# Top-32 attention and two expert stages on one core: mask by clipped distance on ScalarE and one GpSimd subtraction, weight splits on GpSimd

## The reference

```python
top_k = 32
scale = 1.0 / np.sqrt(D)                      # D = 64
scores = scale * np.matmul(q, k.transpose(0, 1, 3, 2))
kth = np.partition(scores, -top_k, axis=-1)[..., -top_k:-top_k + 1]
scores = np.where(scores >= kth, scores, -1000000000.0)
scores = scores - np.max(scores, axis=-1, keepdims=True)
attn = np.exp(scores)
attn = attn / (np.sum(attn, axis=-1, keepdims=True) + 1e-09)
out = np.matmul(attn, v)
...
rms = np.sqrt(np.mean(x * x, axis=-1, keepdims=True) + 1e-06)
xn = x / rms * rms_g
g = xn @ w_gate                               # w_gate, w_val: 512 x 1536
out = (g / (1 + np.exp(-g)) * (xn @ w_val)) @ w_out
```

## Time and profile before

| | us |
|---|---|
| median of 3 runs | 741.94 |
| span of the profiled execution | 741.7 |
| PE busy | 686.1 (93%) |
| DVE busy | 478.9 (65%) |
| ACT busy | 270.4 (36%) |
| POOL busy | 281.5 (38%) |

### The profile page before, as it was taken

One profiled execution on the slowest core, in us unless ns is written; L12 is line 12 of the kernel. 1 busy time (PEld: TensorE's weight loads), 2 busy tenths in 40 slices (PEclk: granted clock), 3 DMA queues, 4 the chain that ended last, 5 costly groups with the idle time before them and its releaser, 6 DMA issues.

```text
span 741.7 us, 10642 instructions
## 1 busy us (share of the span) xinstructions
PE 686.1 (93%) x3862; PEld 557.7 (75%) x3862; DVE 478.9 (65%) x1090; ACT 270.4 (36%) x545; POOL 281.5 (38%) x233
## 2 busy tenths in 40 slices
PE   5696789999999999999999999999994999999994
PEld 3574667588687578688688688687653999999994
DVE  3999979989979968979979979972211011111110
ACT  4385565354354354354354354342210011101110
POOL 1556665646455445545546455452000011110002
PEclk9666599999999999999999999999995999999998
DMA  9999000000000000000000000000055677676501
GB/s 186 363 384 263 0 15 1 0 15 1 14 15 1 15 15 1 11 20 1 14 15 1 15 1 0 15 2 15 0 212 166 256 263 259 231 245 234 204 20 34
DMA packets 52908, 65.43 MB, mean 88 GB/s; under 512 B 32058, under 2 KB 32058, under 8 KB 52860
## 3 DMA queue, kind: packets, MB, share of 16 engines
q1 hardware_dynamic: 51116, 60.05, 25.3%
q0 software_dynamic: 1744, 4.76, 1.7%
HBM read 52.89 MB, written 12.30 MB: 88 GB/s over the span
## 4 chain that ended last, share of the span: by engine, by line
PE 81%; DVE 13%; ACT 1%; DMA 1%; issue 1%; POOL 1%; SPq 0%; POOLq 0%; DVEq 0%; ACTq 0%
PE ps L451 13%; PE ps L593 10%; PE ps L607 10%; PE ps L423 10%; PE ps L401 8%; PE ps L440 6%; PE ps L444 6%; PE ps L441 6%; PE ps L414 4%; PE ps L388 3%; DVE w_top L1006 3%; DVE m L1001 3%; DVE w_parts L909 2%; DVE w_top L993 2%; DVE m L982 1%
## 5 line engine op out<-in xcount | busy, mean ns | idle before, releaser
L1116 POOL TENSOR_SCALAR s_ring<-s_ring,m 128x576 f32<-128x576 f32 x72 | 124.3, 1727 | 179.4 <-DVE m L1010 148.2
L423 PEld LDWEIGHTS ps<-arena,pt_ring 128*128 128x128 f32 (+3 forms) x800 | 99.9, 187 | 22.9 <-issue 8.9
L423 PE MATMUL ps<-arena,pt_ring 128*128 128x65 f32 (+3 forms) x800 | 107.6, 274 | 3.8 <-ACT pt_ring L666 3.7
L1006 DVE MATCH_REPLACE8 w_top<-m,w_top 128x576 f32<-128x576 f32 x144 | 105.8, 742 | 0.0
L1118 POOL TENSOR_TENSOR p_ring<-p_ring,s_ring 128x576 f32<-128x576 f32 x72 | 102.0, 1417 | 6.0
L1001 DVE MAX8 m<-w_top 128x8 f32<-128x576 f32 x144 | 101.6, 747 | 0.0
L451 PE MATMUL ps<-wo_space,hid 128*128 128x512 f32 x216 | 95.8, 593 | 0.0
L401 PE MATMUL ps<-arena,q_cols 128*128 128x288 f32 (+1 forms) x320 | 92.4, 444 | 2.1 <-ACT q_cols L666 1.4
L440 PE MATMUL ps<-w_parts,x_hi 128*128 128x512 f32 x216 | 92.3, 428 | 0.9 <-ACT x_hi L666 0.8
L666 ACT ACTIVATE pt_ring<-ps 128x512 f32<-128x512 f32 (+1 forms) x144 | 54.0, 428 | 95.9 <-PE ps L415 95.6
L441 PE MATMUL ps<-w_parts,x_hi 128*128 128x512 f32 x216 | 85.2, 395 | 0.0
(11 more groups left out here) (116 smaller groups left out, 812.1 us busy)
## 6 DMA issues: line engine op xcount, KB each, us to landing
w_loads<-in_moe_w SPq DMA_DIRECT2D x16, 2048.0 KB, 9.0
dispatched_rows<-hid SPq DMA_DIRECT2D x18, 260.0 KB, 7.4
w_loads<-in_moe_w_gate SPq DMA_DIRECT2D x1, 3072.0 KB, 10.8
w_loads<-in_moe_w_val SPq DMA_DIRECT2D x1, 3072.0 KB, 18.6
wo_space<-in_moe_w_out SPq DMA_DIRECT2D x1, 3072.0 KB, 13.6
arena<-dispatched_rows SPq DMA_DIRECT2D x8, 341.2 KB
out_rows<-hid SPq DMA_DIRECT2D x9, 256.0 KB, 5.2
q_space<-in_q SPq DMA_DIRECT2D x8, 256.0 KB, 2.9
```

The source lines that it names most:

```text
L423: last = mm(ao_ps(u % H, r0, r1), pt_ring[0:n, u % 2, j * P + r0:j * P + r1], vs[b][0:n, j, u % H, :], start=(j == 0), stop=(j == KC - 1))
L1006: vec.match_replace(w_top[:, a, :], m8[:, u % 8, i, :], w_top[:, a, :], NEG).then_inc(s["top_step"], 1)
L1116: gp.tensor_scalar(sc, sc, m8[:, n % 8, TOPK // 8 - 1, 7:8], None, ALU.is_ge).then_inc(s["pchain"], 1)
```

## The change

The exponential moves behind the mask. DVE no longer writes the bias; instead it writes, once per pair and after its last maximum, `far` = the 32nd largest times 2^90. ACT computes relu(far - 2^90 * score): zero where the score is at or above the 32nd largest, and a huge number below it. This is done for both units of a pair in the odd step `u0 + 3`. POOL subtracts it from the score (`lowered`), in one instruction where there were two, and writes the exponential's bias for both units of a pair. ACT takes the exponential in place in step `u + 4`, as the first thing of its step (in slot 4 the second, after `ao`), and that now signals `masked`. The factor 1/8 moves from the exponential to the copy of the queries. All 12 weight pieces now go one way: ACT writes `hi`, and POOL does the two scalings and the subtraction.

The diff, cut to its core (the changed file has other line numbers: its exponential is line 766, its relu 793, `far` 999, the weight multiplies 1100 and the subtraction 1112):

```diff
@@ ffn_block (PE)
-                    if m > in_vec(m):
-                        pe.wait_ge(s["w_lo_set"], m - in_vec(m))
-                    if in_vec(m) > 0:
-                        pe.wait_ge(s["w_lo_vec"], 2 * in_vec(m))
+                    pe.wait_ge(s["w_lo_set"], m)
@@ ACT, after the copy of ao and ahead of turned_probs(u)
+                if 0 <= u < NT * H:
+                    act.wait_ge(s["lowered"], u + 1)
+                    act.wait_ge(s["bias_set"], u // 2 + 1)
+                    nc.scalar.activation(p_ring[:, u % PR, :], p_ring[:, u % PR, :], ACT.Exp,
+                                         bias=nbias[:, u % 8:u % 8 + 1]).then_inc(s["masked"], 1)
@@ ACT, copy of the scores
-                        act.wait_ge(s["masked"], n - SR + 1)
+                        act.wait_ge(s["lowered"], n - SR + 1)
@@ ACT, after the copy of x_hi
-                u = n - EXP_LAG
-                if 0 <= u < NT * H:
-                    act.wait_ge(s["bias_set"], u + 1)
-                    if u >= PR:
-                        act.wait_ge(s["pt_done"], u - PR + 1)
-                    nc.scalar.activation(p_ring[:, u % PR, :], s_ring[:, u % SR, :], ACT.Exp,
-                                         bias=nbias[:, u % 8:u % 8 + 1], scale=SCALE).then_inc(s["exp_done"], 1)
+                for u in (n - 3, n - 2) if n % 2 else ():
+                    if 0 <= u < NT * H:
+                        act.wait_ge(s["far_set"], u // 2 + 1)
+                        if u >= PR:
+                            act.wait_ge(s["pt_done"], u - PR + 1)
+                        nc.scalar.activation(p_ring[:, u % PR, :], s_ring[:, u % SR, :], ACT.Relu, scale=-FAR,
+                                             bias=far[:, u % 2:u % 2 + 1]).then_inc(s["marked"], 1)
@@ ACT, weight pieces
-                    for c in half if m not in VEC_PIECES else ():
-                        nc.scalar.activation(raw[:, c, cols], raw[:, c, cols], ACT.Copy, scale=gain[:, c:c + 1]).then_inc(s["w_scaled"], 1)
@@ DVE, beside(n)
-                if m in VEC_PIECES:
...
-                    for c in half:
-                        vec.scalar_tensor_tensor(out=lo[:, c, cols], in0=raw[:, c, cols], scalar=gain[:, c:c + 1],
-                                                 in1=hi[:, c, cols], op0=ALU.mult, op1=ALU.subtract).then_inc(s["w_lo_vec"], 1)
@@ DVE, pair
-                    vec.tensor_scalar(nbias[:, u % 8:u % 8 + 1], m8[:, u % 8, 0, 0:1], -SCALE, None,
-                                      ALU.mult).then_inc(s["bias_set"], 1)
...
+                dve.wait_ge(s["th_set"], u0 + 2)
+                if u0 > 0:
+                    dve.wait_ge(s["marked"], u0)
+                vec.tensor_scalar(far[:].rearrange("p (a w) -> p a w", w=1), m8[:, u0 % 8:u0 % 8 + 2, TOPK // 8 - 1, 7:8], FAR, None,
+                                  ALU.mult).then_inc(s["far_set"], 1)
@@ POOL
-                if 0 <= m < 4 * FB and m not in VEC_PIECES:
-                    pool.wait_ge(s["w_scaled"], 2 * (m - in_vec(m)) + 2)
+                if 0 <= m < 4 * FB:
+                    pool.wait_ge(s["w_hi_set"], 2 * m + 2)
+                    for c in half:
+                        gp.tensor_scalar(raw[:, c, cols], raw[:, c, cols], gain[:, c:c + 1], None, ALU.mult).then_inc(s["w_scaled"], 1)
+                    pool.wait_ge(s["w_scaled"], 2 * m + 2)
                     gp.tensor_tensor(lo[:, half[0]:half[1] + 1, cols], raw[:, half[0]:half[1] + 1, cols],
                                      hi[:, half[0]:half[1] + 1, cols], ALU.subtract).then_inc(s["w_lo_set"], 1)
+                if n < NT * H and n % 2 == 0:
+                    pool.wait_ge(s["th_set"], n + 2)
+                    gp.tensor_scalar(nbias[:, n % 8:n % 8 + 2].rearrange("p (a w) -> p a w", w=1), m8[:, n % 8:n % 8 + 2, 0, 0:1], -1.0, None,
+                                     ALU.mult).then_inc(s["bias_set"], 1)
                 if n < NT * H:
-                    pool.wait_ge(s["th_set"], n + 1)
-                    pool.wait_ge(s["exp_done"], n + 1)
-                    gp.tensor_scalar(sc, sc, m8[:, n % 8, TOPK // 8 - 1, 7:8], None, ALU.is_ge).then_inc(s["pchain"], 1)
-                    pool.wait_ge(s["pchain"], 4 + n + 1)
-                    gp.tensor_tensor(pr, pr, sc, ALU.mult).then_inc(s["masked"], 1)
+                    pr = p_ring[:, n % PR, :]
+                    pool.wait_ge(s["marked"], n + 1)
+                    gp.tensor_tensor(pr, s_ring[:, n % SR, :], pr, ALU.subtract).then_inc(s["lowered"], 1)
```

More of the change, by code:

```diff
@@ L9 @@
+import math
 from contextlib import ExitStack
@@ L29 @@
 LAG = 4
-EXP_LAG = 2
+FAR = 2.0 ** 90
 KEYS_AT = 3
 SPLIT_AT = 6
-VEC_PIECES = (1, 3, 5, 7, 9, 11)
 RANK = 14
@@ L70, in build @@
     assert B == 2 and NT == 9 and MIX == 4 and H == 8 and KL == 64 and 0 < REST <= P
-    assert S % 2 == 0 and FB == 3 and CF == 12 and CD == 4 and C1 == 8
+    assert S % 2 == 0 and math.frexp(SCALE)[0] == 0.5 and FB == 3 and CF == 12 and CD == 4 and C1 == 8
     disp = nc.dram_tensor("dispatched_rows", [TRASH + N, ROW], F32).ap()
@@ L111, in build @@
         nbias = sb("nbias", [P, 8])
+        far = sb("far", [P, 2])
         rden = sb("rden", [P, H])
@@ L190, in build @@
             "disp_zero out_zero id_set z_set pchain achain vchain "
-            "k_turned k_acted k_veced k1_copied w_hi_set w_scaled w_lo_set w_lo_vec "
+            "k_turned k_acted k_veced k1_copied w_hi_set w_scaled w_lo_set "
             "t_full t_free "
-            "s_done s_copied bias_set top_step th_set exp_done masked pt_done pt_copied pv_done "
+            "s_done s_copied top_step th_set far_set bias_set marked lowered masked pt_done pt_copied pv_done "
             "ao_copied normed x_sum pstep rinv_set x_hi_set blk_full tanh_done silu_done val_done out_full out_copied "
@@ L233, in kind_of @@
             return "mix" if t == MIX else 0 if t < MIX else 1
-        def in_vec(m):
-            return sum(p < m for p in VEC_PIECES)
         def split_piece(m):
@@ L695, in q_columns @@
                 pairs = q_cols[:].rearrange("p (g a) n -> p g a n", a=2)
-                copy(pairs[0:64, :, 0, :], turned[0:64]).then_inc(s["achain"], 1)
+                nc.scalar.activation(pairs[0:64, :, 0, :], turned[0:64], ACT.Copy, scale=SCALE).then_inc(s["achain"], 1)
                 act.wait_ge(s["achain"], t + 1)
-                copy(pairs[64:P, :, 1, :], turned[64:P]).then_inc(s["t_free"], 1)
+                nc.scalar.activation(pairs[64:P, :, 1, :], turned[64:P], ACT.Copy, scale=SCALE).then_inc(s["t_free"], 1)
             def hidden_columns(n):
@@ L810, in _ @@
                         nc.scalar.activation(hi[:, c, cols], raw[:, c, cols], ACT.Copy, scale=gain[:, c:c + 1]).then_inc(s["w_hi_set"], 1)
-                    if m not in VEC_PIECES:
-                        act.wait_ge(s["w_hi_set"], 2 * m + 2)
-                    for c in half if m not in VEC_PIECES else ():
-                        nc.scalar.activation(raw[:, c, cols], raw[:, c, cols], ACT.Copy, scale=gain[:, c:c + 1]).then_inc(s["w_scaled"], 1)
                 dense(n)
@@ L900, in beside @@
             def beside(n):
-                m = n - SPLIT_AT
-                if m in VEC_PIECES:
-                    dve.wait_ge(s["w_hi_set"], 2 * m + 2)
-                    raw, hi, lo, half, cols = split_piece(m)
-                    for c in half:
-                        vec.scalar_tensor_tensor(out=lo[:, c, cols], in0=raw[:, c, cols], scalar=gain[:, c:c + 1],
-                                                 in1=hi[:, c, cols], op0=ALU.mult, op1=ALU.subtract).then_inc(s["w_lo_vec"], 1)
                 t = due(n, VEC_XLO)
@@ L985, in _ @@
                     dve.wait_ge(s["top_step"], done + a + 1)
-                    vec.tensor_scalar(nbias[:, u % 8:u % 8 + 1], m8[:, u % 8, 0, 0:1], -SCALE, None,
-                                      ALU.mult).then_inc(s["bias_set"], 1)
-                for a in range(2):
-                    u = u0 + a
                     if u >= 2:
@@ L1104, in _ @@
                 m = n - SPLIT_AT
-                if 0 <= m < 4 * FB and m not in VEC_PIECES:
-                    pool.wait_ge(s["w_scaled"], 2 * (m - in_vec(m)) + 2)
+                if 0 <= m < 4 * FB:
+                    pool.wait_ge(s["w_hi_set"], 2 * m + 2)
                     raw, hi, lo, half, cols = split_piece(m)
+                    for c in half:
+                        gp.tensor_scalar(raw[:, c, cols], raw[:, c, cols], gain[:, c:c + 1], None, ALU.mult).then_inc(s["w_scaled"], 1)
+                    pool.wait_ge(s["w_scaled"], 2 * m + 2)
                     gp.tensor_tensor(lo[:, half[0]:half[1] + 1, cols], raw[:, half[0]:half[1] + 1, cols],
                                      hi[:, half[0]:half[1] + 1, cols], ALU.subtract).then_inc(s["w_lo_set"], 1)
+                if n < NT * H and n % 2 == 0:
+                    pool.wait_ge(s["th_set"], n + 2)
```

(11 more changed lines are left out.)

## The result

| kernel | median us (runs) | ratio to before [95%] | first output product | a tile |
|---|---|---|---|---|
| before | 741.85 (4) | 1 | 133.0 | 54.0 |
| after | 786.35 (4) | 1.0588 [1.057, 1.0606] | 154.3 | 57.3 |

A forecast was written before the change was run, and what follows sets the result against it. It took PE as the bound from 130 us on and DVE, with PE at a lower clock, before that. 741.9 + 24 (full part) + 11 (early part) = 777 us, range 764 to 792.

The forecast's parts named there:

- Full part: Steps 20 to 75: PE's transposes wait in each tile for the exponential behind ACT's dense instructions, +24 us.
- the holds by slot: Transposes' delay per tile: slot 7 1.75 us, slot 6 0.5, slot 4 0.4, slots 1 and 3 0.3, slot 2 0.2.
- the half microsecond that I had allowed: Slot 6: the dispatch DMA may come 0.5 us sooner, as shorter POOL work lies ahead of it.
- Early part: Before 130 us: POOL's row of all 12 weight pieces delays PE's value block of step 19, +11 us in all.
- dear end of +17: Upper end of the early term, if POOL's multiply takes 1.56 us.
- the 4 I had set: Early stretch: some 4 us in which POOL waits for its relus, within the 84.5 us for its pieces.
- the 8 that I had forecast: PE stands still some 8 us ahead of step 19's value block.
- the 1.5 I had set for the lower clock: After PE's wait ahead of step 19's block, its next products run at the lower clock: +1.5 us.
- The choice within the bounds: POOL's multiply price: 1.3 us taken from the two-input instruction, between 0.5 to 0.7 (fill) and 1.56 (scaled comparison).
- Cheap multiply: Rival, chance 0.19: POOL at 0.6 us a multiply keeps up, early term only +1, 767 us.
- Clock follows: Rival, chance 0.14: slot 7's 1.75 us hold takes PE to the lower clock, adding 8 to 12 us, 787 us.
- Faster: Rival, chance 0.04: transposes stay covered and the early stretch gives back DVE's pieces, 727 us.
- DVE's work: Early stretch: removing DVE's 3.44 us of weight pieces a pair gives nothing back, as POOL's pair takes 13.4 us.

The follow-up runs named there:

- e1: Changed kernel with the exponential of every unit taken a step earlier, at the end of step u+3 ahead of ACT's dense instructions: 767.09 us, ratio 1.0318.
- e2: Changed kernel with the weight pieces shared out as before the change (six on DVE, six scaled on ACT and subtracted on POOL): 774.39 us, ratio 1.0423.
- e6: Kernel before, old mask kept, with all 12 weight pieces multiplied and subtracted on POOL: 771.86 us, ratio 1.0398.
- e8: Changed kernel, weight pieces shared as before, every exponential a step earlier and, in early steps, ahead of ACT's key and weight pieces: 741.33 us, ratio 0.9986.

## Why the prediction was right, and what was mis-sized

- **Direction and mechanism**: right for both parts. Each part is undone by an experiment of its own, e1 and e2, and both together leave 8 of 44.5 us. The two parts of the change overlap in the early stretch and don't add up: the mask part alone (e2) costs 31.8 us over the kernel before, the weight part alone (e6) 29.1, both together 44.5.
- **Full part, +24 forecast, +21.4 measured**: the holds by slot were right to 0.06 us in five of six places. Slot 6 was 0.28 and not 0.5. The dispatch DMA was issued 0.47 us sooner after slot 4 than before (11.45 against 11.92), the half microsecond that I had allowed, and taken off 0.75 it leaves 0.25; I had entered 0.5 in the sum. ACT's output copy now waits for PE's product and no longer for that DMA. Seven tiles at 3.31 would make 23.2, and two of the seven lost less. The last lost 2.8, as it has no slot 4, which the forecast had taken into account. The one at the change of batch (270.59 to 331.88) lost 2.2: there slots 7 and 4 are held by 1.71 and 0.42 us as elsewhere, and slots 6, 1, 2 and 3 by 0.07 at most. The forecast had counted these four slots seven times, and six was right; what covers them there isn't looked into.
- **Early part, +11 forecast, +21.3 measured**: this is the step that was mis-sized, and beyond its own dear end of +17. POOL's first piece was put at 50.2 us and stood at 52.43; its last was put at 134.7 and ended at 145.50. That is 2.2 us for the start and 8.6 in between. Of these, 6.4 are the price of the multiply (24 x 0.265 us) and 4.7 POOL's waits for relus: 4.80, 1.01, 2.19 and 0.74 for the norm, 8.7 us for the 4 I had set. Some 2.5 us come back from terms set a little too long (the eleven subtractions at 1.5 us took 1.39 each from start to start). Then PE's wait ahead of the block, 8.44 us, is the 8 that I had forecast. From the block to the first output product it is 8.7 us after (145.60 to 154.32) and 7.35 before, 1.4 us for the 1.5 I had set for the lower clock. That this is so near is part luck: the block up to the next turn took 4.90 us against 2.88, 2.0 more, and 0.65 came back as the transposes behind it waited 0.25 and not 0.90 us.

ACT's output copy after, where the earlier trace rows have the DMA as its releaser:

```profile
402.82 0.60 ACT L660 ACTIVATE drow<-ps 128x512 f32<-128x512 f32 x1 [4.84 <-PE ps L445]
```

The rows of after, POOL's first and last piece:

```profile
52.43 3.14 POOL L1100 TENSOR_SCALAR w_loads<-w_loads,gain 128x512 f32<-128x512 f32 x2
55.65 2.36 POOL L1102 TENSOR_TENSOR w_parts<-w_loads,w_parts 128x1024 fp32r<-128x1024 f32 x1
...
63.01 1.41 POOL L1112 TENSOR_TENSOR p_ring<-s_ring,p_ring 128x576 f32<-128x576 f32 x1 [4.80 <-ACT p_ring L793]
...
138.59 1.40 POOL L1112 TENSOR_TENSOR p_ring<-s_ring,p_ring 128x576 f32<-128x576 f32 x1 [2.19 <-ACT p_ring L793]
139.97 3.10 POOL L1100 TENSOR_SCALAR w_loads<-w_loads,gain 128x512 f32<-128x512 f32 x2
143.16 2.34 POOL L1102 TENSOR_TENSOR w_parts<-w_loads,w_parts 128x1024 fp32r<-128x1024 f32 x1
```

- **The choice within the bounds**: the scaled comparison had given 1.56 us, and 1.565 is what came. It is the same kind of instruction on the same engine, TENSOR_SCALAR with a column as its scalar. I had preferred the two-input product because it computes the same thing, and that was the wrong nearness.
- **Cheap multiply**: out, at 1565 ns and not 600. Its price was too low as well: it gave ACT's order and the lower clock 1 us of the early stretch, and with the weight pieces shared out as before (e2) 7.8 us stay there. **Clock follows**: out; the window from 372 us, with a hold of slot 7 in it, is at 1.00, and the transposes behind the hold took 0.66 us. **Faster**: not as the change stands, though e8 shows that its mask, rightly placed, is no slower than the old one.
- **DVE's work**: I had forecast that removing it gives nothing back. The trace fits this, though no experiment takes this part alone: with POOL full in its place, DVE waited for scores in the early stretch (waits of DVE from 20 to 150 us; 2.2 us before):

```profile
DVE m L970 <- ACT s_ring L660: 18.3, 8, 3.6
```

## What to carry to other kernels

When an instruction moves behind others in an engine's written order, ask at each step what stands ahead of it and for whom that waits; the holds can be read from the trace of before to a few hundredths of a microsecond. Before giving work to an engine with a low busy share, look at which urgent instruction it will stand in front of. And price an unseen instruction by one of the same kind on the same engine, not by one that computes the same.

## What the runs showed of the hardware

- On GpSimd the one-input instruction with a column as its scalar costs more a column than the two-input one: the comparison had 1727 ns for 576 columns where one column has 243, 2.6 ns a column, and the multiply lies on that line with 1565 for 512; the subtraction has 1416 for 576 and 2367 for 1024, 2.1 ns a column. The Trainium skill's GPSIMD Engine Reference, section 4.1, has one-input work at roughly line rate; the measurement decides, and here it is the slower of the two.
- DVE's weight instruction (two SBUF inputs and a column) took 737 ns at the least and 2903 at the most over the twelve before. The subtraction of a piece on POOL, 2813 ns in the median before, took at most 2414 in the changed kernel, where DVE has no such instruction. The Trainium skill's SBUF — State Buffer, section "Who interferes with whom", has the two exclude each other; the traces agree. (The 3.44 us for two that I had named in the prediction are only 1.72 each and say little; the spread from 737 to 2903 is the evidence.)
- I had not expected that DVE's `far`, a TENSOR_SCALAR on 2 columns, is caught in the same way: 169 ns at the least and 1516 at the most. The longest started at 56.53 us and ended with POOL's subtraction of 55.65 to 58.01. Of the four that took over 0.5 us, three end so, within 0.05 us of the end of a subtraction on POOL; the fourth (71.42 to 72.00) doesn't, and what held it isn't known. From 150 us on none took over 172 ns. The same section names this instruction among those that can take the shared pair of ports when their operands meet its conditions. Line 909 before and line 999 after, each alone (ns least/median/most, first and last start):

```profile
L909 DVE SCALAR_TENSOR_TENSOR w_parts<-w_loads,gain,w_parts x12: 737/746/2903, 49.9 to 124.2; 128x512 fp32r<-128x512 f32 x12
```
```profile
L999 DVE TENSOR_SCALAR far<-m x36: 169/170/1516, 23.9 to 539.3; 128x2 f32<-128x2 f32 x36
```
